# Down weights and block jobs of a two-layer kernel moved between stages

## The reference

```python
sig = 1.0 / (1.0 + np.exp(-f_logit))
f = lower_bound + (1.0 - lower_bound) * sig
for t in range(S):
    h = f[:, t] * h + (1.0 - f[:, t]) * x[:, t]
    y[:, t] = h
# layer 0
h = y @ w_in0
z = (h * (1.0 / (1.0 + np.exp(-1.702 * h)))) @ w_out0
# layer 1
h = z @ w_in1
g = np.where(h >= 1, h, np.where(h <= -1, 0.0, (h + 1) ** 2 / 4))
out = g @ w_out1
```

## Time and profile before

| | |
|---|---|
| median of 3 runs | 1027.06 us (1026.9 to 1027.15) |
| profiled execution | 1029.47 us |
| its span, first to last instruction | 1027.7 us |
| mean granted TensorE clock | 0.995 |
| PE busy | 1010.1 us, 98% |
| DVE, ACT, POOL busy | 707.4, 719.4, 596.5 us |
| transfers | 133.78 MB, mean 130 GB/s |

### The profile page before, as it was taken

One profiled execution on the slowest core, in us unless ns is written; L12 is line 12 of the kernel. 1 busy time (PEld: TensorE's weight loads), 2 busy tenths in 40 slices (PEclk: granted clock), 3 DMA queues, 4 the chain that ended last, 5 costly groups with the idle time before them and its releaser, 6 DMA issues.

```text
span 1027.7 us, 14282 instructions
## 1 busy us (share of the span) xinstructions
PE 1010.1 (98%) x4377; PEld 819.5 (80%) x4377; DVE 707.4 (69%) x985; ACT 719.4 (70%) x1334; POOL 596.5 (58%) x476
## 2 busy tenths in 40 slices
PE   8998999999999999999999999999999999999998
PEld 6986878788777888888888888888888888888887
DVE  7773876566797676678667668765456767667766
ACT  7664867666777677677676767766667777776665
POOL 4576777677687347646536655634664673655331
PEclk9998999999999999999999999999999999999999
DMA  9776543722444432232334232223223233423330
GB/s 311 250 243 243 189 173 135 246 97 88 153 174 138 165 124 97 74 105 72 122 140 149 72 104 76 96 84 125 97 74 106 72 108 111 148 73 105 116 108 39
DMA packets 55453, 133.78 MB, mean 130 GB/s; under 512 B 6224, under 2 KB 19152, under 8 KB 54352
## 3 DMA queue, kind: packets, MB, share of 16 engines
q1 hardware_dynamic: 55232, 132.87, 37.0%
q10 hardware_dynamic: 144, 0.00, 0.0%
HBM read 108.86 MB, written 23.99 MB: 129 GB/s over the span
## 4 chain that ended last, share of the span: by engine, by line
PE 88%; POOL 3%; DMA 3%; issue 2%; ACT 2%; DVE 1%; SPq 0%; ACTq 0%; DVEq 0%; POOLq 0%
PE chain L617 24%; PE acc L676 16%; PE acc L672 16%; PE acc L673 16%; PE pair L617 11%; PE single L617 6%; DMA blocks_kept<-zout 1%; POOL g_lo L1470 1%; DMA zout<-w_in_dram 1%; DMA w_a<-blocks_kept 1%; POOL xin1lo L1438 1%; ACT g_hi L956 0%; POOL raw_more L1418 0%; POOL xin0lo L1438 0%; DVE zout L1182 0%
## 5 line engine op out<-in xcount | busy, mean ns | idle before, releaser
L1470 POOL TENSOR_TENSOR g_lo<-g_act,g_hi 128x512 fp32r<-128x512 f32 (+2 forms) x277 | 367.9, 1330 | 400.9 <-ACT g_hi L956 392.4
L916 ACT ACTIVATE spare<-chain 128x512 f32<-128x512 f32 (+1 forms) x264 | 156.8, 594 | 203.5 <-PE chain L617 196.7
L1227 DVE TENSOR_TENSOR spare<-pair,spare 128x512 f32<-128x512 f32 (+1 forms) x176 | 120.9, 687 | 185.6 <-PE pair L617 185.3
L956 ACT ACTIVATE g_hi<-g_act 128x512 fp32r<-128x512 f32 (+2 forms) x277 | 172.9, 624 | 4.2 <-DVE g_act L1251 3.3
L617 PE MATMUL chain<-xin0hi,w_main 128*128 128x512 f32 (+3 forms) x424 | 163.8, 390 | 8.2 <-DMA w_a<-blocks_kept 4.0
L672 PE MATMUL acc<-g_hi,w_down0hi 128*128 128x512 f32 (+1 forms) x384 | 151.0, 393 | 0.9 <-DVE zraw L1215 0.6
L676 PE MATMUL acc<-g_lo,w_down0hi 128*128 128x512 f32 (+1 forms) x384 | 151.2, 394 | 0.1
L673 PE MATMUL acc<-g_hi,w_down0lo 128*128 128x512 f32 (+1 forms) x384 | 150.8, 393 | 0.0
L676 PE MATMUL acc<-g_lo,w_down1hi 128*128 128x512 f32 (+1 forms) x384 | 150.4, 392 | 0.3 <-POOL g_lo L1470 0.3
L672 PE MATMUL acc<-g_hi,w_down1hi 128*128 128x512 f32 (+1 forms) x384 | 150.0, 391 | 0.3 <-DVE zraw L1215 0.3
L673 PE MATMUL acc<-g_hi,w_down1lo 128*128 128x512 f32 (+1 forms) x384 | 150.0, 391 | 0.0
(11 more groups left out here) (125 smaller groups left out, 1955.4 us busy)
## 6 DMA issues: line engine op xcount, KB each, us to landing
w_main<-sums_kept SPq DMA_DIRECT2D x88, 512.0 KB, 3.6
w_main<-blocks_kept SPq DMA_DIRECT2D x88, 256.0 KB, 3.1
w_a<-blocks_kept SPq DMA_DIRECT2D x88, 128.0 KB, 3.9
sums_kept<-raw_more SPq DMA_DIRECT2D x12, 512.0 KB, 2.9
zout<-w_in_dram SPq DMA_DIRECT2D x20, 256.0 KB, 3.5
out_dram<-zout SPq DMA_DIRECT2D x10, 512.0 KB, 5.6
zraw<-w_out_dram SPq DMA_DIRECT2D x16, 256.0 KB, 5.0
blocks_kept<-w_main SPq DMA_DIRECT2D x8, 512.0 KB, 4.9
```

Of the source, the lines that this page charges most:

```text
L916: act.activation(snap[k][:, 0:n], chain[g % 2][:, 0:n], ACT.Copy).then_inc(s_snap, 1)
L956: act.activation(g_hi[h % 4][:, 0:n], activated(h), ACT.Copy).then_inc(s_ghi, 1)
L1227: dve.tensor_tensor(to[:, 0:n], bank[:, 0:n], snap[(0, 2, 1)[k]][:, 0:n], ALU.add).then_inc(s_evac, 1)
L1470: pool.tensor_tensor(g_lo[h % 4][:, 0:n], g_act[h % 4][:, 0:n], g_hi[h % 4][:, 0:n].bitcast(F32), ALU.subtract).then_inc(s_glo_pool, 1)
```

## The change

It moves work between places; no operation is added or left out.

- `SUMS_AT`: jobs 0 to 2 are now at tiles 1, 5 and 9 of stage 1 (jobs 0 to 3 were at 1, 4, 7 and 10); jobs 3 to 7 at groups 0 to 4 of stage 2 (4 to 7 at 0 to 3); jobs 8 and 9 at groups 5 and 6 of stage 2 (were at 4 and 5). Jobs 10 to 15 keep their groups.
- Down weights of layer 1: groups 0 to 3 at tiles 0, 2, 4, 8 of stage 1 in two buffers; groups 4 to 7 at groups 2, 3, 5, 6 of stage 2 in the other two, loaded by SP at groups 1 and 4 of stage 2.
- `load_gate(3)` is issued one group earlier in stage 1; in stage 1 down loads stand behind the weights; in later stages `kept` stands ahead of `keep_more`.
- For jobs 8 to 15: `more_hi` moves from `fill2` of the group before to `fill1` of its own; `sums_hi` from `fill2` to `fill0` of the next group; `more_lo` from place 0 to place 2 on VectorE, `weight_sums` from place 1 to place 2 on GpSimd.
- In stage 2 the sigmoids, f, drives, scans and input sums of chunk 3 stand in groups 0 to 4 in another order, one to two places earlier.

```diff
 def down_buffer(l, g):
-    return g % 2 if l else g % 4
+    return g % 4 if l == 0 else g % 2 + g // 4 * 2
...
-for _g in range(4):
-    SUMS_AT[1, 3 * _g + 1] = _g
-    SUMS_AT[2, _g] = 4 + _g
+for _g in range(3):
+    SUMS_AT[1, 4 * _g + 1] = _g
+for _g in range(5):
+    SUMS_AT[2, _g] = 3 + _g
...
-DOWN_AT = (0, 2, 4, 6, 8, 13, 14, 15)
+DOWN_AT = (0, 2, 4, 8)
+DOWN_AT_GROUP = (2, 3, 5, 6)
...
-                if si == 1:
-                    if g < 5:
-                        load_raw_down(1, g + 2)
-                    if g == 5:
-                        keep_z(0)
-                    if g == 6:
-                        load_raw_down(1, 7)
-                        load_gate(3)
+                if (si, g) == (1, 5):
+                    keep_z(0)
...
+                if si == 2 and g in (1, 4):
+                    load_raw_down(1, 4 + g // 4 * 2)
+                    load_raw_down(1, 5 + g // 4 * 2)
...
+                if si == 1 and g in (1, 2):
+                    load_raw_down(1, g + 1)
+                if (si, g) == (1, 5):
+                    load_gate(3)
...
             def fill1(si, g):
+                if SUMS_AT.get((si, g), 0) >= NG:
+                    more_hi(SUMS_AT[si, g])
                 if si == 2:
...
+                    if g in DOWN_AT_GROUP:
+                        down_hi(1, 4 + DOWN_AT_GROUP.index(g))
...
             def fill0(si, g):
+                if SUMS_AT.get((si, g - 1), 0) >= NG:
+                    sums_hi(SUMS_AT[si, g - 1])
...
             def fill(si, g, place):
                 l, c = STAGES[si]
-                if place == 0 and SUMS_AT.get((si, g), 0) >= NG:
+                if place == 2 and SUMS_AT.get((si, g), 0) >= NG:
                     more_lo(SUMS_AT[si, g])
                 if si == 2:
...
+                    drives, scans = ((1, 0), (1, 3), (2, 2), (3, 0)), ((1, 2), (2, 0), (2, 3), (3, 1))
...
+                    if place == 1 and g in DOWN_AT_GROUP:
+                        down_lo(1, 4 + DOWN_AT_GROUP.index(g))
```

More of the change, by code:

```diff
@@ L176, in down_before @@
         return (0, g - 4) if g >= 4 else None
-    return (1, g - 2) if g >= 2 else (0, NG - 4 + g)
+    return (1, g - 2) if g % 4 >= 2 else (0, NG - 4 + down_buffer(l, g))
 def down_loads(l, g):
-    return g // 4 + 1 if l == 0 else 2 + g // 2 + 1
+    return g // 4 + 1 if l == 0 else 2 + g % 4 // 2 + 1
 SUMS_AT = {}
+for _g in range(3):
+    SUMS_AT[1, 4 * _g + 1] = _g
+for _g in range(5):
+    SUMS_AT[2, _g] = 3 + _g
+for _g in range(2):
+    SUMS_AT[2, 5 + _g] = NG + _g
+    SUMS_AT[3, _g] = NG + 2 + _g
 for _g in range(4):
-    SUMS_AT[1, 3 * _g + 1] = _g
-    SUMS_AT[2, _g] = 4 + _g
     SUMS_AT[4, _g] = NG + 4 + _g
-for _g in range(2):
-    SUMS_AT[2, 4 + _g] = NG + _g
-    SUMS_AT[3, _g] = NG + 2 + _g
 LATE = {3: 1, 5: 0, 7: 0}
 X_LO_AT = (8, 9, 11, 12, 13, 14, 15)
-DOWN_AT = (0, 2, 4, 6, 8, 13, 14, 15)
+DOWN_AT = (0, 2, 4, 8)
+DOWN_AT_GROUP = (2, 3, 5, 6)
 def by_dve(h):
@@ L997, in fill1 @@
             def fill1(si, g):
+                if SUMS_AT.get((si, g), 0) >= NG:
+                    more_hi(SUMS_AT[si, g])
                 if si == 2:
-                    if g < 4:
-                        sigmoid_step(3, g)
-                    if g == 5:
+                    if g in (0, 2):
+                        sigmoid_step(3, (0, 0, 3)[g])
+                    if g == 1:
+                        f_step(3, 1)
+                    if g in DOWN_AT_GROUP:
+                        down_hi(1, 4 + DOWN_AT_GROUP.index(g))
+                    if g == 4:
                         x_hi(3, T1)
@@ L1012, in fill2 @@
             def fill2(si, g):
-                if (si, g) in SUMS_AT:
+                if SUMS_AT.get((si, g), NG) < NG:
                     sums_hi(SUMS_AT[si, g])
-                following = (si, g + 1) if g + 1 < NG else (si + 1, 0)
-                if SUMS_AT.get(following, 0) >= NG:
-                    more_hi(SUMS_AT[following])
                 if si + 1 == NS:
@@ L1020, in fill2 @@
                 if si == 2:
-                    if g < 4:
-                        f_step(3, g)
-                    if g in (2, 5, 6):
-                        x_hi(3, {2: B21, 5: T3, 6: T4}[g])
+                    if g in (0, 2):
+                        f_step(3, (0, 0, 3)[g])
+                    if g == 1:
+                        sigmoid_step(3, 2)
+                    if g in (2, 4, 5):
+                        x_hi(3, {2: B21, 4: T3, 5: T4}[g])
                 elif STAGES[si + 1][0] == 1:
@@ L1039, in fill0 @@
                 if si == 2:
-                    if g in (2, 5, 6):
-                        x_hi(3, {2: B11, 5: B22, 6: T2}[g])
+                    if g == 1:
+                        sigmoid_step(3, 1)
+                    if g == 2:
+                        f_step(3, 2)
+                    if g in (2, 4, 5):
+                        x_hi(3, {2: B11, 4: B22, 5: T2}[g])
                 elif STAGES[si + 1][0] == 1:
@@ L1302, in fill @@
                 l, c = STAGES[si]
-                if place == 0 and SUMS_AT.get((si, g), 0) >= NG:
+                if place == 2 and SUMS_AT.get((si, g), 0) >= NG:
                     more_lo(SUMS_AT[si, g])
                 if si == 2:
-                    if 1 <= g <= 4 and place == 0:
-                        drive_step(3, g - 1)
-                    if 1 <= g <= 3 and place == 2:
-                        scan_step(3, g - 1)
-                    if (g, place) == (4, 2):
+                    drives, scans = ((1, 0), (1, 3), (2, 2), (3, 0)), ((1, 2), (2, 0), (2, 3), (3, 1))
+                    if (g, place) in drives:
+                        drive_step(3, drives.index((g, place)))
+                    if (g, place) in scans[:3]:
+                        scan_step(3, scans.index((g, place)))
+                    if (g, place) == scans[3]:
                         last_scan(3)
-                    if (g, place) in ((4, 3), (5, 0), (5, 2)):
-                        t_sum(3, {(4, 3): 0, (5, 0): 1, (5, 2): 2}[g, place])
+                    if (g, place) in ((3, 2), (3, 3), (4, 0)):
+                        t_sum(3, {(3, 2): 0, (3, 3): 1, (4, 0): 2}[g, place])
+                    if place == 1 and g in DOWN_AT_GROUP:
+                        down_lo(1, 4 + DOWN_AT_GROUP.index(g))
                 elif l == 0 and c + 1 < CHUNKS:
@@ L1499, in fill @@
                     sums_lo(SUMS_AT[si, g - 1])
-                if place == 1 and (si, g) in SUMS_AT:
+                if (si, g) in SUMS_AT and place == (1 if SUMS_AT[si, g] < NG else 2):
                     weight_sums(SUMS_AT[si, g])
```

9 lines of the change are left out of this document (6 added, 3 removed).

## The result

The changed kernel took 1030.72 us (median of 22 runs, 1028.68 to 1032.59), the kernel before 1028.88 us on the same chips (22 runs, 1026.90 to 1032.91). The ratio is 1.0019, 95% interval 1.0011 to 1.0027: no gain, and 0.2% slower by these runs, where 1.35% faster was forecast. The three runs of before that the forecast was made against lay at the low end of its 22. The profiled run of the changed kernel took 1031.88 us, its span 1030.1 us.

What follows compares the result with a forecast made beforehand. TensorE was taken as the bound, with 17.1 us to win. Terms -6.6 - 4.3 - 2.0 - 3.0 + 2.0 = -13.9 us took the 1027.1 us median to 1013.2 us, range 1009.5 to 1019.5.

Steps and rivals of the forecast that it cites:

- Stage 1 loses four down jobs and a sum job, all beside full windows: nothing.: Stage 1: taking these jobs away changes no time, since TensorE's windows there are full.
- the fifth: Rival: windows stay short because other queues hold ScalarE at the new places; 1027 us, chance 0.04.
- Done at 73.4 + 3.2 + 3.9 = 80.5, at best 79.3: End of stage 1: third sums job, from GpSimd free through sums, remainder, lower half and split, ends at 80.5.
- from about 81.9: Start of stage 2: SP issues its weights from then (slot free), leaving 0.5 us wait; gain 6.6 us.
- Rival 1: Start of stage 2: weights still late, third job holding SP; 3 us stall, 5 us returned, 1018 us, chance 0.14.
- The wait of 1.88 us goes, and with it 4.3.: Stage 2, group 4: raw load issued further ahead of its split ends ScalarE's wait; gain 4.3 us.
- So 2.0 us of stall, in groups 3 and 4.: Stage 2: VectorE's added work and waits make TensorE stall 2.0 us, without a slow clock; bounds 0 and 8.
- slack of 1.5 us: Stage 2: how much later VectorE's copy may run before ScalarE's copy behind it holds TensorE.
- Stage 3, 2.0.: Start of stage 3: ScalarE reaches its wait for a write later than the 3.14 us it stood; gain 2.0 us.
- I take 3.0 of 3.7: Stage 4: the same new order for twelve to fifteen wins 3.0 us, VectorE staying as full.
- what comes in: Stage 2: down jobs moved in and the gate chain pressed into three groups cost 2.0 us.
- Rival 4: Stage 2, groups 2 to 6: VectorE's lateness carried on unpaid, 4.3 us each, slower clock; 1032.7 us, chance 0.03.

Runs made afterwards that it cites:

- a_raw_early: Changed kernel with the loads of down groups 2 and 3 issued early in stage 1, ahead of weights and first job's write: 1026.82 us, ratio 0.9986.
- a_both: Changed kernel with early down loads and stage 2's first weights ahead of the third job's write, raw load and gates: 1021.66 us, ratio 0.9929.
- a_weights_first: Changed kernel with SP issuing stage 2's first weights ahead of the third job's write, raw load and gates: 1025.66 us, ratio 0.9969.
- b_splits: Kernel before with only the new places of the block and sum splits of groups 8 to 15: 1025.94 us, ratio 0.9964.

## Why the prediction was wrong, step by step

**"Stage 1 loses four down jobs and a sum job, all beside full windows: nothing."** This term, put at nothing, failed first and cost 3.8 us. The step counted the work taken away and not the two down loads that were put further back on SP. The diff shows them move from the top of one group's block to the end of the next one's, behind the weights (their wait ends at 55.03) and `kept` (its write goes out at 56.22): 57.05 in place of 47.44. I followed SP's queue at the end of stage 1 and not at its start. Stage 1 had been full, so the cover seemed certain. It was full because those loads were early. No rival held this; the fifth, at 1027, had ScalarE held by other queues, but at the new places of the splits.

**"Done at 73.4 + 3.2 + 3.9 = 80.5, at best 79.3", weights out "from about 81.9".** The job was done at 87.4, and 83.9 even without the lag of stage 1 (a_raw_early). The sum of durations left out that the remainder has a fixed place two tiles later, behind a wait for that tile. 3.5 us of the job's lateness come from the first step, 3.4 from this one. Only the 3.4 count at the start of stage 2: without the lag of stage 1 the weights and TensorE were both 3.5 us earlier, and the stall was the same (2.95 and 2.98). The landing held (6.55 us, or 6.50 in a_raw_early, against 7.30), and so did the time at which the slot is free: with the weights first they went out at 82.25 in a_both (81.9 forecast). So this step is the dearest: the start of stage 2 won 1.0, not 6.6. What held the weights was their place behind the job's write: issued ahead of it, they cost 0.3 (a_weights_first) although the job was as late. Rival 1, weights still late because the third job holds SP, describes what happened here; it had 0.14, its stall of 3 us was 2.98, and its 5 us came out as 6.2.

**Group 4, "The wait of 1.88 us goes, and with it 4.3."** Right, shown by b_splits (4.3 to 0.7) and by the clock of 1.00 in that window. In the changed kernel it can't be seen because the next term fills the same groups.

**"So 2.0 us of stall, in groups 3 and 4."** Mechanism right, size too small. In group 2 VectorE waited 2.17 us at the down remainder (I had 1.8), as said; in group 3 it did not wait (I had 1.0), and in groups 5 and 6 it waited 2.77 us each, which was not covered (1.1 us lost, I had nothing). The remainders themselves took 0.92, 1.31, 0.69 and 1.76 us where I had 0.90 for each; the last section shows why. And TensorE waited for lower halves of hidden values, made by VectorE and GpSimd, and not for ScalarE's copies on whose slack of 1.5 us I had reckoned. In all 5.2 us were lost in groups 2 to 7. Of these 2.3 come with the order of splits (b_splits), which I had counted as free on GpSimd, and 2.9 with the rest of the change in the stage.

**Stage 3, 2.0.** Right: 1.9 to 0 in every kernel with the new order.

**"I take 3.0 of 3.7" in stage 4.** 0.4 came. The releaser that I read before, ScalarE's wait for a write, went, and GpSimd's lower half was late next: GpSimd was busy for 23.36 of 25 us there, more than VectorE, whose row I argued from in the window before it.

Put together, by the table: the forecast had -15.9 and +2.0 us; what came is -3.3 (1.0, 0.4 and 1.9 won) and +3.8, with groups 2 to 7 at +0.9 (4.3 won, 5.2 new) and 1.0 in the start and stage 0, where single profiles of other kernels differ as much. That makes +2.3 to +2.4, and the medians differ by 1.84. Forecast and profiles are 16.3 us apart: 5.6 from the start of stage 2, 3.8 from stage 1, 3.2 from what comes in, 2.6 from stage 4, 1.0 from the start and 0.1 from stage 3. Rival 4, the only one that was slower, did not happen: VectorE's lateness was not carried on, and group 5 lost nothing. The chance of 0.03 for no change and 0.03 for slower was far too small: six terms each rested on what is late next, and I took each of them at its likeliest.

## What to carry to other kernels

Follow every transfer whose place in a queue changes, at the start of a stage as at its end, and ask which wait now stands ahead of it; a stage that is full before the change is full by those places. When the completion of a side job is forecast, read whether its last step has a fixed place in the order, since then it ends when that place comes, however little work it is. If the thing that is late is a weight load, try moving that load alone to the head of its queue before moving work between stages: here it gave 6 of the 7 us in one edit, and the spreading gave nothing measurable.
